# Attention, gated unit and experts in one kernel: attention divided by its row sums after the product with v, and three groups of work moved in the order

## The reference, cut to what matters

```
# attention: 4 batches x 8 heads, 576 rows, head_dim 64
scores = scale * q @ k.T
scores = where(causal, -1e9, scores + minimum(-(cum_i - cum_j), 0))      # cum: running sum of max(s, 0)
attn   = exp(scores - rowmax);  attn = attn / (rowsum(attn) + 1e-9)
x      = concat_heads(attn @ v)                                           # 4 x 576 x 512
# gated unit with token mixing
h = gelu_tanh(x @ w_in);  u, v = halves of h
v_n = (v - mean) / sqrt(var + 1e-6) * g_ln
x   = x + (u * (w_sg @ v_n + b_sg)) @ w_out
# experts: 8, one for each token, routed by logits and a local gate
out[token] = p[e] * (relu(x @ w1[e]) @ w2[e])
```

## Time and profile before

| | us |
|---|---|
| median of three runs (lowest, highest) | 983.89 (983.05, 987.94) |
| the profiled execution | 983.82 |
| its span | 981.80 |

### The profile page before, as it was taken

The page is one execution under the profiler, slowest core; times in us unless marked ns, Lnnn a source line. Parts: engine busy times, 40 slices in busy tenths (PEclk is TensorE's granted clock), DMA queues, the critical chain, the costliest instruction groups (busy, mean ns, idle before and its releaser), DMA issues.

```text
span 981.8 us, 16466 instructions
## 1 busy us (share of the span) xinstructions
PE 837.6 (85%) x5253; PEld 712.9 (73%) x5254; DVE 567.6 (58%) x1219; ACT 380.7 (39%) x862; POOL 379.1 (39%) x481
## 2 busy tenths in 40 slices
PE   2787788799978879979979999946999999999993
PEld 1566667688857768857869868926788888888773
DVE  5578647866547767546777524455664566356221
ACT  2444444533344534344434334123543244334110
POOL 1688646654545664535655430002111111111112
PEclk9989889989999989999989999965999999999997
DMA  4611101011021011020110010066353355330100
GB/s 120 184 39 43 40 13 33 14 32 32 16 79 31 15 33 31 16 79 11 36 25 14 7 49 1 1 244 249 134 207 134 126 196 211 134 124 23 44 34 23
DMA packets 81420, 70.61 MB, mean 72 GB/s; under 512 B 61960, under 2 KB 61960, under 8 KB 81322
## 3 DMA queue, kind: packets, MB, share of 16 engines
q1 hardware_dynamic: 77354, 58.49, 19.2%
q0 software_dynamic: 4000, 11.28, 3.5%
HBM read 59.72 MB, written 11.86 MB: 73 GB/s over the span
## 4 chain that ended last, share of the span: by engine, by line
PE 68%; DVE 12%; POOL 7%; ACT 7%; issue 3%; DMA 1%; POOLq 0%; DVEq 0%; ACTq 0%
PE obank L926 13%; PE sbank L1814 9%; PE sbank L1816 8%; PE sbank L1815 8%; PE sbank L1247 6%; PE sbank L1005 6%; POOL probs L510 4%; PE tbank L994 3%; PE sbank L978 3%; ACT probs L590 2%; DVE nmax L743 2%; PE sbank L980 2%; PE tbank L1005 2%; PE obank L1059 1%; POOL cube L532 1%
## 5 line engine op out<-in xcount | busy, mean ns | idle before, releaser
L510 POOL TENSOR_SCALAR probs<-probs,recip 128x128 f32<-128x128 f32 (+4 forms) x160 | 204.4, 1288 | 176.8 <-DVE recip L753 176.1
L590 ACT ACTIVATE probs<-sbank,nmax 128x128 f32<-128x128 f32 (+4 forms) x160 | 91.2, 570 | 249.2 <-DVE nmax L743 248.8
L978 PE MATMUL sbank<-k,q 128*128 128x256 f32 (+2 forms) x192 | 77.7, 410 | 63.5 <-POOL q L499 54.9
L1610 POOL DMA_INDIRECT out_dram<-y,sid x25 | 25.3, 1011 | 217.9 <-DVE y L1775 214.3
L743 DVE TENSOR_REDUCE nmax<-sbank 128x1 f32<-128x128 f32 (+4 forms) x160 | 84.7, 535 | 41.1 <-PE sbank L985 39.5
L978 PEld LDWEIGHTS sbank<-k,q 128*128 128x128 f32 x192 | 39.8, 207 | 71.8 <-issue 59.6
L994 PE MATMUL tbank<-ident,probs 128*128 128x128 f32 (+2 forms) x480 | 74.5, 278 | 5.9 <-DVE pT L759 5.4
L1005 PE MATMUL sbank<-pT,v_raw 128*64 128x128 f32 x640 | 78.2, 278 | 0.2 <-ACT pT L599 0.2
L1814 PE MATMUL sbank<-w_high,xsT_h 128*128 x184 | 74.9, 407 | 1.9 <-DVE xsT_l L1739 1.7
L1323 DVE TENSOR_TENSOR w_low<-w_low,w_high (+1 forms) x64 | 74.0, 1218 | 0.7 <-ACT w_high L1679 0.3
L1005 PEld LDWEIGHTS sbank<-pT,v_raw 128*64 128x64 f32 x640 | 70.2, 139 | 5.3 <-issue 4.2
(11 more groups left out here) (290 smaller groups left out, 2163.5 us busy)
## 6 DMA issues: line engine op xcount, KB each, us to landing
w_low<-in_moe_w_dram SPq DMA_DIRECT2D x16, 2048.0 KB, 13.3
k_raw<-in_k_dram SPq DMA_DIRECT2D x32, 128.0 KB, 2.3
q_raw<-in_q_dram SPq DMA_DIRECT2D x32, 128.0 KB, 2.4
v_raw<-in_v_dram SPq DMA_DIRECT2D x32, 128.0 KB, 2.2
x_dram<-x SPq DMA_DIRECT2D x4, 1024.0 KB, 4.3
win_raw<-in_moe_w_in_dram SPq DMA_DIRECT2D x1, 2048.0 KB, 10.7
wsg_raw<-in_moe_w_sg_dram SPq DMA_DIRECT2D x1, 1152.0 KB, 6.0
wout_raw<-in_moe_w_out_dram SPq DMA_DIRECT2D x1, 1024.0 KB, 12.8
```

The costliest lines, as they stand in the source:

```text
L510: nc.gpsimd.tensor_scalar(w, w, recip[u][0:r, i:i + 1], None, ALU.mult).then_inc(normed, 1)
L590: nc.scalar.activation(probs_view(u, i, r), score_view(i, r), ACT.Exp, bias=nmax[u][0:r, i:i + 1], accum_out=sums[u][0:r, i:i + 1]).then_i ...
L978: nc.tensor.matmul(dst, q1[u][:, q_cols], k1[u][:, cols], start=True, stop=False)
```

## The change

Five things change in the first half.

1. `norms` and `normed` are gone. `turn_probs` waits for the exponential itself, so the product with v is made of undivided exponentials. `invert` runs once a head, behind the first maximum of the next step, on all five sums. SyncE's `spread_recips` writes the 5 x 128 reciprocals to DRAM, waits for that, and reads them back as a row of 576 numbers in each of 64 partitions (`recipT`). `output` multiplies with `recipT` and waits for it.
2. The pairs of heads 2 to 9 (`early`) are transposed behind scores 1 of the odd head, into the two banks of `obank`, which hold no units there; their first half is copied in mid head.
3. w_sg is transposed in steps 0, 2, 4, 6 and 8.
4. Subtractions move from VectorE to GpSimd (`x_l` 0 to 2, `vn_l` 3 and 4, all `g_l`), and the `vn_h` copies from GpSimd to ScalarE. The mixing and gating on VectorE run one point later, the normalising is spread over three points. The first v unit and the first mixing unit wait for their inputs piece by piece.
5. The last two `x2` tiles of a batch run at the first two points of the next one; `TURN` goes ahead of tile 2. `store_x2` moves one step later. The last batch with units keeps its tiles.

```diff
+            def spread_recips(h):
+                sp.wait_ge(inverted, h + 1)
+                with nc.allow_non_contiguous_dma("small"):
+                    sp.dma_start(recip_dram[h % 2, :].rearrange("(i p) -> p i", p=P),
+                                 recip[h % 2][:, :]).then_inc(recip_out, 16)
+                sp.wait_ge(recip_out, 16 * (h + 1))
+                if h:
+                    sp.wait_ge(out_done, h)
+                sp.dma_start(recipT[:, :], recip_dram[h % 2, 0:S].rearrange("(a n) -> a n", a=1).broadcast_to([D, S])
+                             ).then_inc(recip_in, 16)
...
             for t in range(HEADS + 1):
+                if t:
+                    spread_recips(t - 1)
                 if t % 2 == 0 and t // 2 + 1 < PAIRS:
...
-                pe.wait_ge(normed, ST * h + i + 1)
+                pe.wait_ge(exped, ST * h + i + 1)
...
                 dve.wait_ge(av_part, h + 1)
-                nc.vector.tensor_copy(dst[own_rows[h % 2], MAIN], O[TOP, :]).then_inc(out_part, 1)
+                dve.wait_ge(recip_in, 16 * (h + 1))
+                nc.vector.tensor_tensor(dst[own_rows[h % 2], MAIN], O[TOP, :], recipT[:, MAIN],
+                                        ALU.mult).then_inc(out_part, 1)
...
+        def early(p):
+            return 1 <= p and 2 * p - 1 <= HPB
+        def k_bank(p):
+            return obank[:, 0, :] if early(p) else tbank[:, 1, :]
+        def q_bank(p):
+            return obank[:, 1, :] if early(p) else O
...
-        def units_at(p):
-            if p < POINTS - 3:
-                return [p]
-            first = POINTS - 3
-            return {first: [LOGITS, LOGITS + 1], first + 1: [TILES, TILES + 1, TILES + 2],
-                    first + 2: [TILES + 3, TILES + 4, TURN]}[p]
+        def units_at(b, p):
+            here = [(b, p)] if p <= LOGITS - 1 else []
+            if p < 2 and b:
+                here.append((b - 1, TILES + 3 + p))
+            if p == POINTS - 3:
+                here = [(b, LOGITS), (b, LOGITS + 1)]
+            if p == POINTS - 2:
+                here = [(b, TILES), (b, TILES + 1)]
+            if p == POINTS - 1:
+                here = [(b, TURN), (b, TILES + 2)]
+                if b == B - 2:
+                    here += [(b, TILES + 3), (b, TILES + 4)]
+            return here
...
+                    for kk in range(KT):
+                        if n == 0 and kk < KT - 1:
+                            pe.wait_ge(xl_pool, (KT - 1) * b + kk + 1)
+                        elif n == 0:
+                            pe.wait_ge(xl_done, b + 1)
...
+                    for kk in range(ST):
+                        if n == MIX and kk < 3:
+                            pe.wait_ge(m_vnl, 3 * b + kk + 1)
+                        elif n == MIX:
+                            pe.wait_ge(m_vnl_pool, 2 * b + kk - 2)
```

More of the change, by code:

```diff
@@ L501, in twice, with fill @@
                 pool.wait_ge(kq_twice, 4 * p + u + (1 if cols == MAIN else 3))
[L503 to L512, removed]
+            def fill(t, k, latest):
                 if point_of(t, k) is None:
@@ L532, in fill @@
                     nc.gpsimd.tensor_tensor(c, x, x, ALU.mult).then_inc(squared, 1)
[L533 to L537, removed]
-                        nc.gpsimd.tensor_copy(vn_h[:, m, :], vn[:, m, :]).then_inc(m_vnh, 1)
+                    latest = squared, done + 1
@@ new lines, in _ @@
+                if this and even:
+                    pool.wait_ge(*latest)
+                    twice(t // 2, 0, TAIL, 5)
+                    twice(t // 2, 1, TAIL, 5)
+                if first_x:
+                    latest = x_low(t // HPB - 1, 0)
+                latest = fill(t, 1, latest)
+                if first_x:
+                    latest = x_low(t // HPB - 1, 1)
+                latest = fill(t, 2, latest)
+                if first_x:
+                    latest = x_low(t // HPB - 1, 2)
@@ L670, in _ @@
                     exps(t, 2)
+                    if not even and early((t + 1) // 2):
+                        pair_main((t + 1) // 2, 0)
                 fill(t, 1)
@@ L680, in _ @@
                     fill(t, 3)
-                    if t + 1 < HEADS:
+                    if t + 1 < HEADS and not early((t + 1) // 2):
                         pair_main((t + 1) // 2, 0)
@@ L827, in fill @@
                     if p in (11, 12):
[L828 removed]
+                        for m in ((0,), (1, 2))[p - 11]:
                             dve.wait_ge(m_vnh, ST * b + m + 1)
@@ L898, in _ @@
                     row_max(t, 3)
+                if not even and early((t + 1) // 2):
+                    pair_k((t + 1) // 2, 0)
+                    pair_q((t + 1) // 2, 0)
                 if before:
@@ L1095, in fill @@
                     pe.wait_ge(misc_in, 48)
-                for n in units_at(p):
-                    unit(b, n)
+                for x in units_at(b, p):
+                    unit(*x)
             pe.wait_ge(pool_own, 5)
@@ L1120, in _ @@
                             pe.wait_ge(out_done, h)
-                    elif this:
+                    elif this and not early(t // 2):
                         pe.wait_ge(kq_low, 5 * (t // 2) + 3)
```

211 lines of the change are left out of this document (114 added, 97 removed).

## The result

The changed kernel takes 1050.78 us (median; 1048.45 to 1051.93) where the kernel before takes 983.89: a ratio of 1.0668, 95% interval 1.0633 to 1.0704. It is 6.7% slower; the forecast was 941. The profiled execution took 1051.62 us, with a span of 1049.8 and a granted clock of 0.922.

What follows compares the result with a forecast made beforehand. The order in which engines wait for each other bounds attention, chiefly GpSimd's normalisation ahead of its k and q copies. Terms sum to 48.8 us, less 6 for small waits, net 43: 983.8 to 941 us, range 925 to 963.

Steps and rivals of the forecast that it cites:

- the size of the trip: Reciprocals to DRAM and back before `output`: 5.5 us, between 5.2 and 7.0, covered in every head at 5.5.
- the prediction's own rival: Late reciprocals: a 12 us trip makes heads wait at `output`, 81 us lost against 43 won, 1022 us; chance 0.06.
- Normalisation and `output`: GpSimd loses 204.4 us of normalisation; the division in `output` costs nothing, 0.68 us like the copy.
- Startup: Head 1: TensorE waits 5.5 us for the loads of heads 2 and 3, transposed earlier now; a loss of 4.5 us.
- Light handovers: Handover to a new pair in the light heads: tail transposes 1.9 us sooner, 4 x 2 = 8 us gained.
- Head 11 to 12: In each of three batches, handover and mixing unit end at 196.5 instead of 203.1: 6.5 x 3 = 19.5 us gained.
- head 9 to 10: Without normalisation ahead of GpSimd's k and q copies the 2.2 us gap goes in three batches: 8.1 us gained in all.
- batch end: Two `x2` tiles move on, TensorE's 4.0 us wait becomes about 1; 3.8 us with half clock, twice: 7.6 gained.
- exponentials: TensorE's waits on exponentials shrink by 0.4 us in each batch, 1.2 us gained in all.
- small waits: Small waits exposed when large ones go: 0.25 us in each of 24 heads with units, 6 us lost.
- First unit: A batch's first unit waits for `x_l` piece by piece: 4.8 us gained in batch 0, 2.05 each in batches 1 and 2.
- the prediction's sign: Forecast is wrong if TensorE still idles over 45 us in the stages that answer to the three attention stretches shown.

Runs made afterwards that it cites:

- e2: Changed kernel with the reciprocals written in 128 pieces of 20 bytes instead of 640 of 4, output off: 961.17 us, ratio 0.9783.
- x1: Changed kernel with the division done by matmuls with a diagonal matrix in place of the transposes, no trip: 999.22 us, ratio 1.0114.
- x3: x1 with the pairs of heads 2 to 8 transposed at the end of the odd head, as in the kernel before: 996.57 us, ratio 1.0095.
- e1: Changed kernel without the trip: both DMAs removed, `recipT` set to one once, division left out: 950.65 us, ratio 0.9652.
- f3: Changed kernel writing one column of reciprocals, 128 pieces of 4 bytes 20 bytes apart, the row read back from an input: 940.62 us, one run.
- x2: x1 with SyncE's start reordered: w_sg loads ahead of a wait, second pair of k and q ahead of the experts' weights: 986.84 us.
- x5: Changed kernel with 128 pieces of 20 bytes written, read at a stride of five, and x2's start order, result whole: 952.31 us, ratio 0.9675.

## Why the prediction was wrong

*The step that failed* is the size of the trip. It was bounded by 5.2 and 7.0 us and taken as 5.5. Measured are 8.3 us to the write's completion and 4.1 from the read's issue to its landing, and with the issues 13 us in all. Both bounds were of another kind. The lower one is a load: its 512 pieces of 4 bytes touch in DRAM too (`w_local` is one column of 512 numbers), but at the side that is read, and land in 2.3 us, while here the touching pieces are written. The upper one is a large write with long rows, which says nothing of small touching pieces. I took them for a bracket since one had small pieces and the other was a write; the row with both didn't exist, and then the bound should have been open above. With the trip at 13 us the prediction's own rival applies: priced at 12 us it gave 1022, decided from 10.4, and had a chance of 0.06. Its price for 12 us was 81 us lost; the trip of some 13 us cost 100.

*The rule of the skill.* The Trainium skill (DMA: Bandwidth & Descriptors, Rules for kernel authors) has one descriptor for each element here, and by that the write is dear. The runs agree only in part: 640 touching pieces wait 8.3 us and 128 touching ones 6.6, so that number is 1.7 us of it. The same page (Anatomy of one DMA) says, of DMAs that GpSimd issues, that most of a DMA's fixed cost is waiting for completion, above all when the target is HBM (the chip's DRAM). The windows of the touching writes, which SyncE issues, agree in kind: a microsecond of work, then silence. The price isn't a fixed one: the prediction's estimate from the page's 2.0 us, some 4 us for the trip, stands against a median of 12.8 from the last reciprocal to the landing, and 5.1 in e2.

*Normalisation and `output`*: right. The two-input instruction takes 683 ns as the copy did, and GpSimd is off TensorE's path but for the start and head 11 to 12.

*Startup*: booked at +4.5. The changed kernel has gaps of 4.3 us on `wsg_raw` and 4.3 on the raw q where before had one of 4.0, and x1 reaches the first tails 4.3 us behind x3. For the pair's loads that is right. The wait on `wsg_raw` was not in the sum; all in all the first tails come 6.2 us (e1) and 4.0 us (f3) later than before (45.70). With the diagonal x2 takes the cost away; with a trip (x5) it comes back as the first trip's wait.

*Light handovers*: booked 2 for each. 1.9 by x1 against x3, but the whole time shows none of it (x3 is no slower than x1). In kernels without the diagonal it hangs on the clock: three pairs of heads take 72.1 us before, 72.9 in e1 and 67.9 in f3, and from 50 to 70 us e1 is granted 0.74, f3 0.91. Why the one has more spells at half clock than the other, with nearly the same waits, is open.

*Head 11 to 12*: forecast a gap of about 2 us and one of 2 inside the mixing unit. In e1, without the late trip, TensorE waits 1.6 us there for GpSimd's q (189.63 to 191.25), and 1.6 and 1.0 inside the unit for VectorE's `vn_l`. From one batch's first unit to the next are 141.3 and 140.3 us, where before had 154.1 and 150.8: 12.7 and 10.5 us gained a batch. The terms of a batch (first unit 2.05, head 9 to 10 2.7, head 11 to 12 6.5, batch end 3.8, exponentials 0.4, less 2 of small waits) make 13.4. Right in kind and somewhat large in size. The wait on `x2` is 1.1 us for the forecast 1, at TensorE's transposes of `logT`.

*First unit*: in e1 no wait above 0.3 us is left in it, where the forecast left 1.5, and it runs at clock 1.00.

*The sum.* Forecast for a trip that is hidden: 43 us. With no trip or a short one the last attention comes 25.6 (e1), 32.1 (x5), 34.1 (e2) and 36.1 us (f3) sooner than before; by e1's median the time is 33 less. So the rest of the sum was too large by 7 to 17 us, spread over the batches and the clock in the light heads; at its best the mechanism gave 84% of the 43. TensorE idles 41.8 us in e1's three stages, under the 45 of the prediction's sign. All of it was turned round by one term, the one that no row showed.

## What to carry to other kernels

A step that no row of the trace shows has no upper bound from rows of another kind: here a load of small touching pieces didn't price a write of them. Ask what the slack is that the whole chain hangs on (here 5.5 to 8.4 us in a light head), and at what price it decides, before trusting the middle of a bracket. A trip of a few numbers through DRAM can be had for about 5 us, if each partition's numbers stay together at the writing side and the strided order is left to the reader on the chip.

## What the runs showed of the hardware

- The completion of a small write to DRAM hangs on how close its pieces lie: 128 pieces of 4 bytes complete in 6.6 us when they touch, 2.7 us at 8 bytes, 1.4 at 20, 1.3 at 64; 640 touching pieces in 8.3. The DMA engines are shown busy for about a microsecond of that.
- VectorE's reciprocal of 64x512 takes 3359 ns, where a multiplication of that shape takes 683; of 64x64, 559 against 217.
- An f32 matmul of a tile is two instructions of 286 ns in the mean over this kernel's shapes, a transpose of it one of 276; 480 tiles keep TensorE busy for 140.5 and 73.6 us.
- A 64x512 multiplication on VectorE with one operand read at a stride of five takes 1080 ns instead of 683.
- In x5, a small write issued behind large loads, with the DMA engines busy (0.97 or more in each window from 29 to 37 us), waited 9.9 us for its completion, where the later ones waited 1.3.
